# Three late tiles instead of four, part of the first ahead of the last split, and rounding work moved between engines

## The chip, the cores and the metric
The kernel runs on one core of a Trainium2 chip. The time is the device time of one execution in microseconds, the median of several runs. Lower is better.

## The reference, cut to what matters
```python
# 1. decayed linear attention over r, k, v (2 x 8 x 768 x 48), y -> x of 1536 tokens x 384
cur = einsum(u * kt, vt); y[t] = rt . (state + cur); state = w * state + einsum(kt, vt)
# 2. mixture of 8 experts, capacity 384, tokens kept in their order
expert_idx = argmax(x @ w_gate)                  # one expert for each token
disp[e, counts[e]] = x[i]; counts[e] += 1        # only while counts[e] < capacity
out[i] = gate_w[i] * (relu(disp @ w1[e]) @ w2[e])[pos[i]]
# 3. h = out @ w_in; softmax-weighted h, layer norm over 1024, @ w_out
```
All of it is float32. Products are made of parts: an operand is rounded to a high part (fp32r) and the remainder is its low part, so `w1_hi`, `w1_lo`, `xe_hi`, `xe_lo` exist beside the raw values.

## The kernel before, in words
The work is cut into tiles of 128 tokens, 12 of them (`NT`). A loop over the tiles does the attention; each turn t also splits tile t-1 into rows of x and logits (`split_x`, `take_logits`, `take_x`), picks each token's expert (`pick_experts`) and counts the tokens of each expert ahead of it (`count_before`), from which a slot in the table `x_slots` in DRAM follows (`place_tokens`). The tiles are picked in groups (`GROUPS`): 0-2, 3-5, 6-7, and then 8, 9, 10 and 11 alone. GpSimd scatters the rows of a tile to their slots with an indirect DMA (`scatter`, L566).

The first expert's rows are wanted before the last tiles could go through DRAM. So the tiles in `LATE` (8 to 11 before) are placed by TensorE: a 0/1 matrix `columns_of` says which token of the tile stands in which of the 224 slots of expert 0 (`rank_late`, `late_columns`, L1125 to L1137), and `place_late` (L1575) multiplies the tile's rows with it, three products of 224 columns, one for each third c of the 384 features, into three PSUM banks. The scattered tiles' rows of expert 0 are read back by SyncE (`load_rows(0, 0)`, L471, once all scatters of the tiles ahead of `LATE[0]` have landed) and turned into the same banks by `place_first_rows` (L1583). From the banks ScalarE rounds `xe_hi` (`act_first_xe_hi`) and VectorE takes the remainder `xe_lo` (`dve_first_xe_lo`, L963). Then the eight experts follow: `pe_up` (w1, eight blocks f, each needs its quarter of `w1_hi` and `w1_lo`), `pe_down` (w2), and between them sums and roundings of h on ScalarE and VectorE (L738, L969, L745, L976). After them come the last two matrix products with the norm.

The engines run in parallel and meet in semaphores; each works through its own list in the order in which the code issues it, and the code's order is written by hand. VectorE's list around the change is, in words: the end of the tile loop, counts and columns of the late tiles, quarters 1 and 2 of `w1_lo` (`lo_w1`, L522), `xe_lo`, and then L1199 to L1226, some fifteen small steps that find each token's place in the output (`sorted_to`). Only after them comes the first sum of h (L969). Quarter 3 of `w1_lo` is GpSimd's (L650), which waits for `sorted_ready` (L1226) first.

GpSimd's loop has, in each turn t, `last_keys(t + 1)` (L589), the decayed state (L619), `own_parts(t + 1)` (L577, L581) and then up to two scatters. VectorE's `add_own` (L1036) waits for `own_parts`.

Of the kernel before, what the change touches and what calls it, by code (L numbers as in the profile page):

```python
# [13 lines left out]
P = 128  # L14


def decay_attention_moe_solu(nc, r, k, v, w, u, w_gate, w1, w2, w_in, w_out, g_ln, out, CAP, N1):
# [27 lines left out]
    with ExitStack() as ctx:  # L45
# [107 lines left out]

        LATE = [NT - 4, NT - 3, NT - 2, NT - 1]
        columns_of = h[:].rearrange("p f n -> p (f n)")[:, 0:len(LATE) * N1].rearrange("p (t n) -> p t n", t=len(LATE))
# [261 lines left out]
        def _(sp):  # L417
# [14 lines left out]
            def load_first_w1(a):  # L432
                rows = slice(a, a + 1)
                sp.dma_start(w1_raw[:, 0, rows], w1_v[0][:, rows]).then_inc(usual.w1_in[0], 16)
# [16 lines left out]
            load_tile(9)  # L451
            load_first_w1(0)
            load_tile(10)
            load_first_w1(1)
            load_tile(11)
            load_first_w1(2)
            load_w2(0, 0)
# [75 lines left out]
        def _(pool):  # L533
# [73 lines left out]
            for t in range(1, NT):  # L607
# [18 lines left out]
                for _ in range(2):  # L626
                    if t >= GROUPS[group_of(stored)][-1] + 4:
                        if stored == 0:
                            pool.wait_ge(slots_zeroed, 16 * E)
                        scatter(stored)  # L630
                        stored += 1
# [116 lines left out]
        def _(act):  # L748
# [64 lines left out]
            for t in range(NT):  # L813
                if t > 0:
                    take_y(t - 1)
                    put_diagonal(t, 1)

                if t == NC:
                    take_k(t + 1)
                if t > 0:  # L820
                    take_x(t - 1)
                if t < NT - 1:
                    if t != NC:
                        take_k(t + 1)
                    put_diagonal(t + 1, 0)
                for n, g in enumerate(GROUPS):
                    if t == g[-1] + 2:
                        gate_exp(n)
                if t >= NT - 2:
                    act_w1_hi(act, 0, usual.w1_in[0], w1_loads(0, 1), usual.w1_hi, parts=[t - NT + 2])  # L830
            take_last_y()
            gate_exp(len(GROUPS) - 2)
            act_w1_hi(act, 0, usual.w1_in[0], w1_loads(0, 1), usual.w1_hi, parts=[2])
            take_x(NT - 1)
            act_w1_hi(act, 0, usual.w1_in[0], w1_loads(0, 1), usual.w1_hi, parts=[3])
            gate_exp(len(GROUPS) - 1)
            act_w2_hi(act, 0, usual.w2_in[0], 16, usual.w2_hi, parts=[0, 1])
            act_first_xe_hi(act)
            act_w2_hi(act, 0, usual.w2_in[0], 16, usual.w2_hi, parts=[2])

# [145 lines left out]
        def _(dve):  # L986
# [169 lines left out]
            for t in range(NT):  # L1156
# [15 lines left out]
                for n, g in enumerate(GROUPS):  # L1172
                    if t == g[-1] + 1:
                        pick_experts(n)
                    if t == g[-1] + 2:
                        if g[-1] in LATE:
                            rank_late(LATE.index(g[-1]))
                        else:
                            place_tokens(n)
                        add_picked(n)  # L1180
                        if g[-1] == LATE[0]:
                            late_columns(0)
            late_columns(1)
            rank_late(2)
            add_picked(len(GROUPS) - 2)
            take_logits(NT - 1)
            pick_experts(len(GROUPS) - 1)
            late_columns(2)
            rank_late(3)
            late_columns(3)  # L1190
            below_max(NT - 1)
            late_slots()
            add_picked(len(GROUPS) - 1)

            lo_w1(dve, 0, 0, usual, parts=[1, 2])
            dve_first_xe_lo(dve)

# [253 lines left out]
        def _(pe):  # L1451
# [122 lines left out]

            def place_late(j):  # L1575

                pe.wait_ge(columns_ready, j + 1)
                pe.wait_ge(x_ready, LATE[j] + 1)
                for c in range(KD):
                    pe.matmul(first_turned(c), x_rows(LATE[j])[:, c * P:(c + 1) * P], columns_of[:, j].bitcast(F32),  # L1580
                              start=(j == 0), stop=False, skip_group_check=True)

            def place_first_rows():  # L1583

                for m in range(usual.tiles):
                    pe.wait_ge(usual.rows_loaded[0][m], 16)
                for c in range(KD):
                    for m, rows in enumerate(usual.rows):
                        last = pe.matmul(first_turned(c)[:, m * P:m * P + rows], rows_in[0:rows, 0, m, c * P:(c + 1) * P],
                                         ident[0:rows, 0:rows], start=False, stop=(m == 1), skip_group_check=True)  # L1590
                    last.then_inc(usual.xe_turned, 1)

# [11 lines left out]
            for t in range(NT):  # L1604
# [8 lines left out]
                for n, g in enumerate(GROUPS):  # L1613
                    if t == g[-1] + 2:
                        count_before(n)
                chunk_out(b, t, c)
            count_before(len(GROUPS) - 2)
            split_x(NT - 1)
            place_late(0)
            place_late(1)  # L1620
            count_before(len(GROUPS) - 1)
            place_late(2)
            place_late(3)
            place_first_rows()
            pe.wait_ge(sum_ready, len(GROUPS))
# [117 lines left out]
```

## Time and profile before
| | us |
|---|---|
| time, median of 3 runs (lowest, highest) | 328.25 (327.98, 329.58) |
| the profiled execution's own time | 328.55 |
| its span, from first to last instruction | 326.8 |
| TensorE busy in it | 312.0 (95%) |
| VectorE busy | 212.2 (65%) |
| ScalarE busy | 196.1 (60%) |
| GpSimd busy | 188.5 (58%) |

The span has three parts: the attention with its tile loop up to about 74 us, the eight experts up to about 206 us, and the norm with the output. The change touches the end of the first and the start of the second. Durations below come from the profiled execution. Matmul records of float32 come in pairs (two passes), so three products of `place_late` are six records.

### The profile page before, as it was taken

The page shows a single profiled execution, that of the slowest core. Times are in us where ns is not written, and L with a number is a line of the kernel's source. Part 1 is how long each engine was busy: PE and PEld are TensorE (multiplying, and loading weights), DVE is VectorE, ACT ScalarE, POOL GpSimd, SP SyncE. Part 2 cuts the span into 40 slices and gives each one's busy share as a digit, 9 for nine tenths or more (in the row PEclk, how much of TensorE's full clock was granted, in tenths as well). Part 3 has the DMA queues.
Part 4 walks back from the last instruction along what each step waited for, and adds up shares of the span by engine and source line. Part 5 has one row for each costly group of instructions (what it writes and reads, how often), then busy time and mean ns, then how long its engine had stood idle before and what let it go on. Part 6 is the DMA issues. An engine that isn't in the chain of part 4 may idle for free.

```text
span 326.8 us, 6597 instructions
## 1 busy us (share of the span) xinstructions
PE 312.0 (95%) x2384; PEld 282.1 (86%) x2384; DVE 212.2 (65%) x489; ACT 196.1 (60%) x375; POOL 188.5 (58%) x170
## 2 busy tenths in 40 slices
PE   6799999989999999999999999999999999999991
PEld 3588888878999999999999999888999999999991
DVE  6856777897765647464555546898987676655610
ACT  2377786877667676676676767466565544543520
POOL 5985688761798898989898969501031101111221
PEclk9999999999999999999999999999999999999997
DMA  8999999971498949485757576000010000000010
GB/s 138 153 245 241 217 195 231 318 281 49 151 386 300 330 136 311 148 284 177 252 196 235 202 228 248 3 1 1 2 48 12 14 24 26 24 25 26 24 48 28
DMA packets 61650, 48.68 MB, mean 149 GB/s; under 512 B 42544, under 2 KB 57008, under 8 KB 61616
## 3 DMA queue, kind: packets, MB, share of 16 engines
q1 hardware_dynamic: 57856, 43.28, 46.0%
q0 software_dynamic: 1920, 4.73, 4.0%
q10 hardware_dynamic: 1840, 0.21, 0.9%
q8 instruction: 21, 0.34, 0.5%
q14 instruction: 13, 0.11, 0.1%
HBM read 38.37 MB, written 9.85 MB: 148 GB/s over the span
## 4 chain that ended last, share of the span: by engine, by line
PE 81%; DVE 6%; ACT 5%; issue 3%; DMA 1%; POOL 1%; DVEq 0%; ACTq 0%; POOLq 0%
PE ps L1391 24%; PE ps L1674 15%; PE ps L1657 15%; PE ps L1392 11%; PE ps L1683 3%; ACT scores L778 3%; PE ps L1527 2%; PE ps L1549 2%; PE ps L1495 2%; PE ps L1580 1%; DMA u_all<-in_u_dram 1%; PE ps L1464 1%; PE ps L1385 1%; PE ps L1522 1%; DVE scores L1054 1%
## 5 line engine op out<-in xcount | busy, mean ns | idle before, releaser
L522 POOL TENSOR_TENSOR w_lo<-w_raw,w_hi 128x768 fp32r<-128x768 f32 x33 | 60.5, 1860 | 9.9 <-DVE w_lo L528 9.8
L1391 PE MATMUL ps<-h,w_hi 128*128 128x448 f32 x192 | 61.8, 378 | 0.2 <-ACT h L745 0.2
L1391 PE MATMUL ps<-xe,w_hi 128*128 128x448 f32 x192 | 61.7, 377 | 0.3
L1674 PE MATMUL ps<-w_hi,h 128*128 128x384 f32 x192 | 51.4, 339 | 0.0
L1392 PE MATMUL ps<-xe,w_lo 128*128 128x224 f32 x192 | 50.7, 264 | 0.0
L1392 PE MATMUL ps<-h,w_lo 128*128 128x224 f32 x192 | 50.7, 264 | 0.0
L684 POOL TENSOR_TENSOR rstd<-var_b,minus_half 128x1 f32<-128x1 f32 x12 | 6.8, 565 | 71.3 <-DVE var_b L1337 71.3
L1657 PE MATMUL ps<-w_hi,xe 128*128 128x512 f32 x144 | 46.5, 392 | 0.2 <-DVE xe L1229 0.2
L969 DVE TENSOR_TENSOR ps<-ps,rk_in 128x448 f32<-128x448 f32 x32 | 20.2, 633 | 32.9 <-ACT rk_in L738 32.6
L1391 PEld LDWEIGHTS ps<-xe,w_hi 128*128 128x128 f32 x192 | 36.0, 188 | 5.0 <-issue 2.3
L528 POOL TENSOR_TENSOR w_lo<-w_raw,w_hi 128x1024 fp32r<-128x1024 f32 x16 | 38.2, 2408 | 1.5 <-DVE w_lo L528 1.5
L1391 PEld LDWEIGHTS ps<-h,w_hi 128*128 128x128 f32 x192 | 36.0, 188 | 3.1 <-ACT h L745 0.5
L1392 PEld LDWEIGHTS ps<-h,w_lo 128*128 128x128 f32 x192 | 36.6, 191 | 0.0
L1392 PEld LDWEIGHTS ps<-xe,w_lo 128*128 128x128 f32 x192 | 36.6, 191 | 0.0
L1674 PEld LDWEIGHTS ps<-w_hi,h 128*128 128x128 f32 x192 | 34.9, 188 | 0.0
L1657 PEld LDWEIGHTS ps<-w_hi,xe 128*128 128x128 f32 x144 | 27.0, 188 | 6.2 <-issue 0.7
L778 ACT ACTIVATE scores<-ident,own 128x128 f32<-128x128 f32 x92 | 29.3, 390 | 4.8 <-DVE own L1036 4.1
L1674 PE MATMUL ps<-w_lo,h 128*128 128x384 f32 x96 | 32.1, 335 | 0.0
L734 ACT ACTIVATE w_hi<-w_raw 128x1024 fp32r<-128x1024 f32 x24 | 24.6, 1055 | 8.6 <-PE ps L1392 7.3
L728 ACT ACTIVATE w_hi<-w_raw 128x768 fp32r<-128x768 f32 x36 | 29.4, 839 | 0.0
L1657 PE MATMUL ps<-w_lo,xe 128*128 128x512 f32 x72 | 28.1, 391 | 0.0
L745 ACT ACTIVATE h<-ps 128x448 fp32r<-128x448 f32 x32 | 17.4, 545 | 16.9 <-DVE ps L969 16.2
(166 smaller groups left out, 621.6 us busy)
## 6 DMA issues: line engine op xcount, KB each, us to landing
w_raw<-in_moe_w_dram SPq DMA_DIRECT2D x15, 1536.0 KB, 8.8
x_slots<-zeros SPq DMA_DIRECT2D x8, 336.0 KB, 4.3
rk_in<-in_r_dram SPq DMA_DIRECT2D x12, 192.0 KB, 4.4
rk_in<-in_k_dram SPq DMA_DIRECT2D x12, 192.0 KB, 4.8
v_in<-in_v_dram SPq DMA_DIRECT2D x12, 192.0 KB, 4.9
out_dram<-zeros SPq DMA_DIRECT2D x1, 2304.0 KB, 8.1
w_raw<-in_moe_w_dram SPq DMA_DIRECT2D x3, 512.0 KB
rows_in<-x_slots SPq DMA_DIRECT2D x8, 192.0 KB, 7.6
```

The source lines that it names most:

```text
L522: eng.tensor_tensor(w1_lo[:, :, cols], w1_raw[:, i, :, cols], w1_hi[:, :, cols].bitcast(F32), ALU.subtract).then_inc(g.w1_lo, 1)
L528: eng.tensor_tensor(w2_lo[:, :, cols], w2_raw[:, i, :, cols], w2_hi[:, :, cols].bitcast(F32), ALU.subtract).then_inc(g.w2_lo if d == 0 els ...
L728: act.activation(w1_hi[:, :, cols], w1_raw[:, i, :, cols], ACT.Copy).then_inc(hi_sem, 1)
L734: act.activation(w2_hi[:, :, cols], w2_raw[:, i, :, cols], ACT.Copy).then_inc(hi_sem, 1)
L745: act.activation(hi[:, 2 * j:2 * j + 2], first_sums(j, n), ACT.Relu).then_inc(g.h_hi, 1)
L778: last = act.activation(scores[:, t % 2, a, p, :], ident[:], ACT.Copy, scale=own[:, 2 * p + a:2 * p + a + 1])
L969: dve.tensor_tensor(first_sums(j, g.n), first_sums(j, g.n), h_rest[:, j % 2, :, 0:g.n], ALU.add)\
L1391: pe.matmul(ps[:, bank, 0:2 * n], w_hi, x[:, c, 0:2 * n], start=first, stop=False, skip_group_check=True)
L1392: return pe.matmul(ps[:, bank, 0:n], w_lo, x[:, c, 0:n], start=False, stop=last, skip_group_check=True)
L1657: last = pe.matmul(hidden_banks(t)[:, a, :], xt[:, c, i * P:(i + 1) * P], wt[:, c, a * 512:(a + 1) * 512], start=(c == 0 and z == 0), stop ...
L1674: last = pe.matmul(ps[:, OB + i, 0:DM], ht[:, f, i * P:(i + 1) * P], wt[:, f, :], start=(f == 0 and z == 0), stop=(f == KF - 1 and z == 2))
L1683: last = pe.transpose(ps[:, TB + f // 4, (f % 4) * P:(f % 4 + 1) * P], solu[i][:, f * P:(f + 1) * P], ident[:])
```

## The change
`LATE` loses tile 8, which is scattered like the ones ahead of it. To keep its scatter from coming too late, GpSimd scatters the tiles from 3 on one turn earlier. On TensorE two of the three products of the first late tile (now 9) stand ahead of the last count and `split_x(11)`; the third product and the rows from DRAM stand behind `split_x(11)`, and the last count and tiles 10 and 11 after them; so the last product into each bank is now one of `place_late(2)`, which releases `xe_hi`. On ScalarE the roundings of w1 and w2 change places with other work. On VectorE `late_columns` and `pick_experts` are reordered, `xe_lo` stands ahead of the two quarters of `w1_lo`, and `below_max(11)` behind them. SyncE issues thirds 1 and 2 of expert 0's w1 ahead of the loads of tiles 10 and 11.

```diff
-        LATE = [NT - 4, NT - 3, NT - 2, NT - 1]
+        LATE = [NT - 3, NT - 2, NT - 1]
@@ sync
             load_first_w1(0)
+            load_first_w1(1)
             load_tile(10)
-            load_first_w1(1)
+            load_first_w1(2)
             load_tile(11)
-            load_first_w1(2)
@@ gpsimd, in the tile loop
-                    if t >= GROUPS[group_of(stored)][-1] + 4:
+                    if stored < LATE[0] and t >= GROUPS[group_of(stored)][-1] + (3 if stored >= 3 else 4):
@@ scalar, in the tile loop: ahead of take_x, not at the turn's end
+                if t >= NT - 2:
+                    act_w1_hi(act, 0, usual.w1_in[0], w1_loads(0, 1), usual.w1_hi, parts=[t - NT + 2])
...
@@ scalar, behind the loop
+            act_w2_hi(act, 0, usual.w2_in[0], 16, usual.w2_hi, parts=[0])
+            act_first_xe_hi(act)
+            act_w2_hi(act, 0, usual.w2_in[0], 16, usual.w2_hi, parts=[1, 2])
             gate_exp(len(GROUPS) - 1)
-            act_w2_hi(act, 0, usual.w2_in[0], 16, usual.w2_hi, parts=[0, 1])
-            act_first_xe_hi(act)
-            act_w2_hi(act, 0, usual.w2_in[0], 16, usual.w2_hi, parts=[2])
@@ vector
-                    if t == g[-1] + 1:
+                    if t == g[-1] + 1 and t < NT - 1:
                         pick_experts(n)
...
+            pick_experts(len(GROUPS) - 2)
+            rank_late(1)
+            add_picked(len(GROUPS) - 2)
             late_columns(1)
...
-
+            dve_first_xe_lo(dve)
             lo_w1(dve, 0, 0, usual, parts=[1, 2])
-            dve_first_xe_lo(dve)
+            below_max(NT - 1)
@@ tensor
-            def place_late(j):
+            def place_late(j, parts=range(KD)):
...
+
+            place_late(0, range(2))
             count_before(len(GROUPS) - 2)
             split_x(NT - 1)
-            place_late(0)
+            place_late(0, range(2, KD))
+            place_first_rows()
+            count_before(len(GROUPS) - 1)
             place_late(1)
-            count_before(len(GROUPS) - 1)
             place_late(2)
-            place_late(3)
-            place_first_rows()
```

TensorE, from the end of the tile loop to the first expert, before. L1565/L1567 are the counts, L1549 `split_x`, L1580 `place_late`, L1589 the rows from DRAM:

```order
L1565 MATMUL ps<-picked,tri_bf 128x8 [waits picked_ready,state_ready,late_rank,sum_ready]
L1549 MATMUL ps<-pick_pair,yt 128x104 [waits x_ready,even_pairs_ready]
L1580 MATMUL ps<-h,w_raw 128x224 [waits x_ready,columns_ready]
L1580 MATMUL ps<-h,w_raw 128x224 x2
L1565 MATMUL ps<-picked,tri_bf 128x8 [waits picked_ready,state_ready,late_rank,sum_ready]
L1580 MATMUL ps<-h,w_raw 128x224 [waits x_ready,columns_ready]
L1580 MATMUL ps<-h,w_raw 128x224 x2
L1589 MATMUL ps<-ident,rows_in 128x128 [waits usual_rows_loaded01,usual_rows_loaded00]
L1627 MATMUL ps<-picked_sum,ones_bf 128x8 [waits late_rank,sum_ready]
```

And of the change (L1563 is the count, L1547 `split_x`, L1578 `place_late`):

```order
L1578 MATMUL ps<-h,w_raw 128x224 [waits x_ready,columns_ready]
L1578 MATMUL ps<-h,w_raw 128x224
L1563 MATMUL ps<-picked,tri_bf 128x8 [waits picked_ready,state_ready,late_rank,sum_ready]
L1547 MATMUL ps<-pick_pair,yt 128x104 [waits x_ready,even_pairs_ready]
L1578 MATMUL ps<-h,w_raw 128x224 [waits x_ready,columns_ready]
L1589 MATMUL ps<-ident,rows_in 128x128 [waits usual_rows_loaded01,usual_rows_loaded00]
L1563 MATMUL ps<-picked,tri_bf 128x8 [waits picked_ready,state_ready,late_rank,sum_ready]
L1578 MATMUL ps<-h,w_raw 128x224 [waits x_ready,columns_ready]
L1578 MATMUL ps<-h,w_raw 128x224 x2
L1627 MATMUL ps<-picked_sum,ones_bf 128x8 [waits late_rank,sum_ready]
```

Two products now stand ahead of the count, and one late tile is gone: before, two tiles stood on each side of the second count, each as a pair of rows (rows that only repeat are left out).

VectorE, just ahead of the steps that find each token's place (L522 is `w1_lo`, L963 `xe_lo`, L1075 `below_max`):

```order
+L963 TENSOR_TENSOR xe<-ps,xe 128x224 [waits usual_xe_hi] x3
+L522 TENSOR_TENSOR w_lo<-w_raw,w_hi 128x3x256 [waits usual_w1_hi] x2
 L1075 TENSOR_SCALAR below<-logits,lmax 128x8
-L1141 TENSOR_SCALAR slot_b<-rank 128x4
-L1143 SCALAR_TENSOR_TENSOR slot<-slot_a,slot_b 128x4 [waits late_slot_a]
-L1151 TENSOR_REDUCE picked_sum<-picked 128x8 [waits counts_done,picked_ready]
-L522 TENSOR_TENSOR w_lo<-w_raw,w_hi 128x3x256 [waits usual_w1_hi] x2
-L963 TENSOR_TENSOR xe<-ps,xe 128x224 [waits usual_xe_hi] x3
-L1199 TENSOR_SCALAR kept<-ps 128x8 [waits total_done]
```

The two quarters of `w1_lo` change sides with `xe_lo`; L1199 is the first step of the chain to `sorted_to`, which now follows L1075.

GpSimd, turns 8 to 10 of the tile loop (L566 is a scatter):

```order
+L566 DMA x_slots<-place,slot 3072x384 [waits x_ready,slot_ready] x2
 L589 TENSOR_TENSOR place<-rk_in,wlast 128x8x48 [waits update_done,k_turned,loaded2]
 L619 TENSOR_TENSOR place<-place,wsq 128x256 [waits y_done,state_ready]
 L577 TENSOR_TENSOR own_place<-rk_in,u_all 128x384 [waits own_step,loaded2,picked_ready]
 L581 TENSOR_TENSOR own_place<-own_place,rk_in 128x384 [waits own_ready,own_step]
-L566 DMA x_slots<-place,slot 3072x384 [waits x_ready,slot_ready] x2
+L566 DMA x_slots<-place,slot 3072x384 [waits x_ready,slot_ready]
```

The scatters of tiles 3 and 4 now stand ahead of the work for tile 10, and one scatter (tile 5) stands where two did.

## Rows read from the trace of the kernel before
**Rows 1.** The page, part 1: busy time, share of the span.
```profile
PE 312.0 (95%) x2384; PEld 282.1 (86%) x2384; DVE 212.2 (65%) x489; ACT 196.1 (60%) x375; POOL 188.5 (58%) x170
```
**Rows 2.** Busy time by stretch, PE alone: window, PE busy (records), clock, DMA share, GB/s.
```profile
74.20:81.40 7.20, 7.17 (x48) 1.00 0.15 47
81.40:90.30 8.90, 8.64 (x53) 1.00 0.48 155
90.30:205.00 114.70, 114.45 (x735) 1.00 0.71 244
```
**Rows 3.** Chain that ended last: start us, us, what.
```profile
84.17 0.55 ACT rk_in L738
...
89.71 0.52 ACT h L745
...
90.31 0.44 PE ps L1391
```
**Rows 4.** Timeline, PE: start us, us, engine line op, tiles, count [idle before].
```profile
74.22 1.14 PE L1549 MATMUL ps<-pick_pair,yt 128*128 128x104 f32 x8
75.20 2.46 PE L1580 MATMUL ps<-h,w_raw 128*128 128x224 f32 x12
...
77.55 2.52 PE L1580 MATMUL ps<-h,w_raw 128*128 128x224 f32 x12
79.90 1.47 PE L1589 MATMUL ps<-ident,rows_in 128*128 128x128 f32 x12
81.21 0.17 PE L1627 MATMUL ps<-picked_sum,ones_bf 128*128 128x8 bf16 x1
```
**Rows 5.** Timeline, DVE, end of the routing.
```profile
79.24 1.84 DVE L522 TENSOR_TENSOR w_lo<-w_raw,w_hi 128x768 fp32r<-128x768 f32 x2
...
82.11 0.16 DVE L1199 TENSOR_SCALAR kept<-ps 128x8 f32<-128x8 f32 x1
...
83.37 0.44 DVE L1217 TENSOR_SCALAR token<-expsum 128x12 f32<-128x12 f32 x1
...
84.36 0.17 DVE L1226 TENSOR_TENSOR sorted_to<-place_a,place_c 128x12 int32<-128x12 f32 x1
84.82 0.63 DVE L969 TENSOR_TENSOR ps<-ps,rk_in 128x448 f32<-128x448 f32 x1 [0.29 <-issue]
```
**Rows 6.** Timeline, POOL, turn 9 on.
```profile
58.61 1.01 POOL L577 TENSOR_TENSOR own_place<-rk_in,u_all 128x384 f32<-128x384 f32 x1 [0.73 <-DVE picked L1103]
59.70 1.01 POOL L581 TENSOR_TENSOR own_place<-own_place,rk_in 128x384 f32<-128x384 f32 x1
60.85 1.01 POOL L566 DMA_INDIRECT x_slots<-place,slot  x1
62.16 0.98 POOL L566 DMA_INDIRECT x_slots<-place,slot  x1 [0.30 <-issue]
...
70.51 0.97 POOL L566 DMA_INDIRECT x_slots<-w_raw,slot  x1 [0.30 <-issue]
...
85.09 1.89 POOL L522 TENSOR_TENSOR w_lo<-w_raw,w_hi 128x768 fp32r<-128x768 f32 x1
```
**Rows 7.** Timeline, DVE, turns 10 and 11.
```profile
61.80 0.55 DVE L1036 TENSOR_REDUCE own<-own_place 128x8 f32<-128x384 f32 x1
...
63.61 0.83 DVE L1084 SCALAR_TENSOR_TENSOR lscore<-logits,lmax,desc 128x8 f32<-128x8 f32 x1
...
72.94 0.23 DVE L1084 SCALAR_TENSOR_TENSOR lscore<-logits,lmax,desc 128x8 f32<-128x8 f32 x1
```
**Rows 8.** Timeline, the queue of SyncE.
```profile
73.12 14.41 SPq L466 DMA_DIRECT2D rows_in<-x_slots  x4
```
**Rows 9.** DMA issues of 70 to 86 us: count, KB each, us to landing.
```profile
rows_in<-x_slots SPq DMA_DIRECT2D x1, 192.0 KB, 2.5
```
**Rows 10.** Timeline, ACT, turn 10 (w1_hi, then the last y but one).
```profile
69.22 0.83 ACT L728 ACTIVATE w_hi<-w_raw 128x768 fp32r<-128x768 f32 x1
69.95 0.57 ACT L791 ACTIVATE yt<-ps 128x512 f32<-128x512 f32 x1
```

More of the change, by code:

```diff
@@ L828, in _ @@
                         gate_exp(n)
-                if t >= NT - 2:
-                    act_w1_hi(act, 0, usual.w1_in[0], w1_loads(0, 1), usual.w1_hi, parts=[t - NT + 2])
             take_last_y()
@@ L1177, in _ @@
                             rank_late(LATE.index(g[-1]))
+                            late_columns(LATE.index(g[-1]))
                         else:
@@ L1180, in _ @@
                         add_picked(n)
-                        if g[-1] == LATE[0]:
-                            late_columns(0)
+            pick_experts(len(GROUPS) - 2)
+            rank_late(1)
+            add_picked(len(GROUPS) - 2)
             late_columns(1)
-            rank_late(2)
-            add_picked(len(GROUPS) - 2)
             take_logits(NT - 1)
             pick_experts(len(GROUPS) - 1)
+            rank_late(2)
             late_columns(2)
-            rank_late(3)
-            late_columns(3)
-            below_max(NT - 1)
             late_slots()
             add_picked(len(GROUPS) - 1)
+            dve_first_xe_lo(dve)
             lo_w1(dve, 0, 0, usual, parts=[1, 2])
-            dve_first_xe_lo(dve)
+            below_max(NT - 1)
             dve.wait_ge(total_done, 1)
@@ L1573, in count_before @@
                 last.then_inc(counts_done, 1)
-            def place_late(j):
+            def place_late(j, parts=range(KD)):
                 pe.wait_ge(columns_ready, j + 1)
                 pe.wait_ge(x_ready, LATE[j] + 1)
-                for c in range(KD):
-                    pe.matmul(first_turned(c), x_rows(LATE[j])[:, c * P:(c + 1) * P], columns_of[:, j].bitcast(F32),
-                              start=(j == 0), stop=False, skip_group_check=True)
+                for c in parts:
+                    last = pe.matmul(first_turned(c), x_rows(LATE[j])[:, c * P:(c + 1) * P], columns_of[:, j].bitcast(F32),
+                                     start=(j == 0), stop=(j == len(LATE) - 1), skip_group_check=True)
+                    if j == len(LATE) - 1:
+                        last.then_inc(usual.xe_turned, 1)
             def place_first_rows():
@@ L1588, in place_first_rows @@
                     for m, rows in enumerate(usual.rows):
-                        last = pe.matmul(first_turned(c)[:, m * P:m * P + rows], rows_in[0:rows, 0, m, c * P:(c + 1) * P],
-                                         ident[0:rows, 0:rows], start=False, stop=(m == 1), skip_group_check=True)
-                    last.then_inc(usual.xe_turned, 1)
+                        pe.matmul(first_turned(c)[:, m * P:m * P + rows], rows_in[0:rows, 0, m, c * P:(c + 1) * P],
+                                  ident[0:rows, 0:rows], start=False, stop=False, skip_group_check=True)
             pe.wait_ge(zero_ready, 1)
```

## The prediction
> **What bounds the kernel now.** I read the page's busy times first: TensorE is busy for 312.0 of 326.8 us [rows 1]. Then the busy time by stretch: from 74.2 to 81.4 us TensorE is busy for 7.17 of 7.20 us, from 90.3 to 205 for 114.45 of 114.70 [rows 2]. Work taken off its list in the first stretch shortens the kernel if nothing else is late. In between, from 81.4 to 90.3 us, the chain of waits leaves TensorE: it runs over ScalarE's L738 at 84.17, VectorE, ScalarE's L745 at 89.71, and is back on TensorE only at 90.31, in the middle of the first `pe_down` [rows 3]. The reader is to see that TensorE is full on both sides of this, while the chain between is one of VectorE and ScalarE. From 90.31 on I let a shift pass through unchanged. So the question is when the first sum of h (L969, at 84.82 [rows 5]) starts, not when `pe_up` does: from L969 to TensorE's row at 90.31 it is 5.49 us, in an order that the change does not touch.
>
> **TensorE's list.** The 24 records of `place_late` take 77.49 - 75.20 = 2.29 us for two tiles and 79.90 - 77.55 = 2.35 for the other two [rows 4] (the count sits at 77.49), 0.19 a record. A tile is 6 records, 1.16 us: removed. Two thirds of the next, 4 records, 0.77 us: moved ahead of `split_x(11)`. Together 1.93 us less between `split_x(11)`, at 74.22, and L1627, at 81.21 [rows 4]. The moved records stand where TensorE waited for little: its last row of the loop ends near 73.7, so they end near 74.5 and `split_x(11)` slips by some 0.3 us, if the loop ends when it did.
>
> **What happens ahead of it.** ScalarE's rounding of a quarter of w1 goes from 69.22, right ahead of the y at 69.95 for which TensorE waits [rows 10], to a place where ScalarE waits for logits. That takes up to 0.73 us out of one wait. But GpSimd's list changes too. The scatters of tiles 3 and 4 (60.85 and 62.16, two that take 2.45 us with the gaps [rows 6]) now stand ahead of the work for tile 10. GpSimd ran without a gap up to there, but L577 waited 0.73 us for the picks, to 58.61 [rows 6]. So it is 2.45 - 0.73 = 1.7 us late, and L581, over at 60.71, is over at 62.4. VectorE's L1036, which waits for it, began at 61.80 [rows 7]. It waits 0.6 us, and for three quarters of a turn VectorE's list has no slack. Of these 0.6 us a part returns: one row of L1084 takes 0.83 us and a later one 0.23 [rows 7], the first beside a GpSimd operation, and the columns of the first late tile leave turn 10. The next turn I put at +0.1 us. With the 0.3 above, `split_x(11)` starts at about 74.65, +0.43 us.
>
> A sentence from the Trainium skill, SBUF — State Buffer, section Who interferes with whom: VectorE and GpSimd share one port pair, an exclusive lock, and whoever starts first holds it for its whole instruction. The long L1084 agrees. By that rule the sum would move with every new overlap, in both directions, by at most one such row at a time, and I change nothing for it.
>
> **The scatter of tile 8 and the rows.** The last scatter ahead of the rows began at 70.51 [rows 6], and the rows were issued at 73.12 [rows 8], each landing in 2.5 us [rows 9]: about 75.6 and 76.0. Now the queue on GpSimd is one scatter longer but begins a turn earlier; I count L581 of tile 11 ending at 67.5, two scatters, the state, and tile 8's scatter at 70.8: +0.3, rows in at 76.3. TensorE reaches them at 74.65 + 0.98 (L1549) + 0.38 (the third product) = 76.0, where it used to reach them at 79.90 [rows 4]. Cover of 3.9 us is gone; what is left is a wait of 0 to 0.3 us, I take 0.1. The wait stands ahead of the last count and both last tiles, so all of it would count.
>
> Then L1627 comes at 81.21 + 0.43 - 1.93 + 0.10 = 79.8. `pe_up` can start about 1.4 us earlier. Its fillers: the columns of the last tile are ready at about `split_x(11)` + 3.8 us and TensorE is there at + 3.9.
>
> **VectorE's list, where the gain goes.** Before, `w1_lo` (two of 0.92 us, 79.24 to 81.08) ran while the rows were turned, and `xe_lo` followed, done at 82.11 when L1199 began [rows 5]. Now `xe_lo` comes first and VectorE idles until `xe_hi` is there. `xe_lo` ends at 82.11 - 1.40 + 0.1 (the last record is one of 224 columns) = 80.8. Behind it come 1.84 us of `w1_lo` and 0.1 of `below_max`, then L1199 to L1226, which took 84.53 - 82.11 = 2.42 us. In them L1217 took 0.44 us beside a scatter [rows 5]; the late scatters are one fewer and start as early, so they should be over by 83, and I take 0.28 off: 2.14. L969 may start at 80.8 + 1.84 + 0.1 + 2.14 + 0.05 = 84.95, against 84.82. Without that credit it is 85.2, with no shift of `split_x(11)` 84.5.
>
> So L969 moves by +0.15 us (-0.3 to +0.8), although `pe_up` starts 1.4 us sooner. TensorE gives its lead back twice: at block 6, whose `w1_lo` is GpSimd's row of 1.89 us (85.09 before [rows 6]) and again waits for `sorted_ready`, now due at 84.9, so that block 6 can start at 86.85 and not at about 85.9; and in `pe_down`, at 90.45.
>
> SyncE's order costs nothing: w1's thirds come sooner, the loads of tiles 10 and 11 wait behind 0.5 MB each, and they have over 5 us until use. ScalarE's two quarters of w2 behind `xe_hi` (about 2.0 us) end at 82.5, ahead of its first row of h at 84.17 before [rows 3]; were they late, VectorE would not notice before 84.5. The exp of tile 11 waits for `below_max`, at 82.8, done before it is read.
>
> **Sum.** The profiled execution took 328.55 us, 326.8 of span and 1.75 around it; +0.15 makes 328.7. The median before is 0.3 below that execution, so I say 328.4.
>
> **The rivals.**
> *The lead survives* (faster in tendency). If the time were set by TensorE's list and not by L969, -1.93 + 0.43 + 0.1 = -1.4 us: 326.9. For it speaks that TensorE is full from 74 to 81. Against it that the chain leaves TensorE at 84.17, and VectorE's 1.94 us of rounding and comparing now stand directly in that chain. Chance 0.14.
> *The earlier scatters cost nothing upstream.* If GpSimd keeps up in turn 9, or VectorE catches up, `split_x(11)` starts at 74.2, L969 at 84.5, -0.3: 328.0. For it: ScalarE's move takes 0.73 us out of a wait on the same way. Chance 0.22.
> *The rows land late* (slower). The one mechanism: TensorE stands at the first row from DRAM. Place: behind the third product of tile 9. Every microsecond that they land after 76.0 is a microsecond of the end. The point from which it makes the kernel slower than before is a landing about 0.1 us later than I assume, and it leaves the band of 0.5% at about 1.5 us. One more scatter turn (1.31 us) on GpSimd, or SyncE's issue slipping behind an unfinished scatter, gives +1.3 on my +0.15: 329.7; a landing twice as slow as the 2.5 us gives +2.5: 330.9. Against it: the scatters queued are as many per stretch. Chance 0.14.
> *The forecast itself*, L969 bound, +0.15: chance 0.50, its own range 328.0 to 329.0.
>
> **Range and chances.** A measurement of this kernel can tell about 0.5%, 1.6 us, from no change: faster is under 326.6, slower over 329.9. The range takes in the surviving lead and the late rows up to one scatter: 326.9 to 329.8. Faster 0.06, same 0.86, slower 0.08.
>
> **What would show it.** In the changed profile: TensorE's first L1391 row about 1.4 us earlier, near 80.2; a wait of VectorE ahead of `xe_lo`; TensorE idle for 0.7 to 1 us at block 6 of the first `pe_up`, and for about 1 us in the first `pe_down`; L969 within 0.5 us of 84.82. L1036 of tile 10 waiting for L581 shows the upstream step, TensorE's wait at L1589 the rows. I am wrong if L969 comes before 84 or if TensorE stands more than 0.5 us at L1589.

## The result, and the profile after

| | median of 6 | lowest to highest | profiled execution (span) |
|---|---|---|---|
| before | 328.21 us | 327.98 to 329.58 | 328.55 (326.8) |
| changed | 329.90 us | 329.46 to 330.44 | 329.46 (327.6) |

The ratio is 1.0047, with an interval of 1.0028 to 1.0066. The kernel became slower by more than the runs scatter, and by slightly less than the 0.5% that the forecast called no change. I had forecast 328.4, with a range of 326.9 to 329.8: the median lies 0.1 us above the range, and the ratio applied to the 328.25 from which I had worked, 329.8, at its upper edge.

Part 1 of the page of the changed kernel (busy time, share, records), then the busy time of TensorE in three stretches that answer to [rows 2] (window, busy, clock, DMA share, GB/s):

```profile
PE 312.1 (95%) x2376; PEld 281.4 (86%) x2378; DVE 211.1 (64%) x490; ACT 196.4 (60%) x375; POOL 188.5 (58%) x170
```
```profile
74.20:81.20 7.00, 6.55 (x46) 1.00 0.17 53
81.20:90.30 9.10, 8.45 (x52) 1.00 0.43 135
90.30:205.00 114.70, 113.82 (x731) 1.00 0.71 243
```

The clock granted to TensorE is full (1.00, 2.4 GHz) in all three, as before, so the clock is no part of the difference between these two profiles. TensorE now idles 0.45 us ahead of the first expert where it idled 0.03, 0.65 in the next stretch where it idled 0.26, and 0.88 in the third where it idled 0.25. The timeline of TensorE shows both places (start us, us, line, tiles, count, idle before; L1563 counts, L1547 is `split_x`, L1578 `place_late`, L1389 and L1390 the products of an expert):

```profile
73.19 1.09 PE L1525 MATMUL ps<-scores,v_in 128*64 128x128 f32 x16 [1.10 <-DVE scores L1054]
74.21 1.02 PE L1578 MATMUL ps<-h,w_raw 128*128 128x224 f32 x4
...
75.23 1.11 PE L1547 MATMUL ps<-pick_pair,yt 128*128 128x104 f32 x8
76.18 0.56 PE L1578 MATMUL ps<-h,w_raw 128*128 128x224 f32 x2
77.00 1.55 PE L1589 MATMUL ps<-ident,rows_in 128*128 128x128 f32 x12 [0.25 <-DMA rows_in<-x_slots]
...
78.44 2.52 PE L1578 MATMUL ps<-h,w_raw 128*128 128x224 f32 x12
80.79 0.17 PE L1627 MATMUL ps<-picked_sum,ones_bf 128*128 128x8 bf16 x1
81.16 0.44 PE L1389 MATMUL ps<-xe,w_hi 128*128 128x448 f32 x1 [0.20 <-DVE xe L963]
...
87.81 0.44 PE L1389 MATMUL ps<-xe,w_hi 128*128 128x448 f32 x1 [0.65 <-POOL w_lo L522]
...
91.19 0.44 PE L1389 MATMUL ps<-h,w_hi 128*128 128x448 f32 x1 [0.65 <-ACT h L745]
```

`pe_up` starts at 81.16, half a microsecond ahead of before (81.66), and `split_x(11)` at 75.23, a microsecond behind [rows 4]. The lead is lost at block 6 (87.81), and the first `pe_down` waits as well. The chain of waits says through what the time ran (start us, us, what):

```profile
70.92 2.62 DMA x_slots<-w_raw,slot
73.56 0.34 SPq L466
...
73.94 2.92 DMA rows_in<-x_slots
...
77.00 1.55 PE ps L1589 x12
78.58 1.63 PE ps L1578 x8
80.23 0.36 ACT xe L722
80.62 1.15 DVE xe L963 x3
81.77 1.73 DVE w_lo L522 x2
...
85.71 0.64 DVE ps L969
```

Before, the chain came from TensorE's list and left it only at 84.17 [rows 3]. Now it comes from the last scatter and the rows from DRAM, crosses TensorE, and is on VectorE from 80.62 on. L969 starts at 85.71, against 84.82 [rows 5].

**A yardstick.** GpSimd's last store of the output, in the changed kernel:

```profile
321.61 0.97 POOL L688 DMA_INDIRECT out_dram<-v_in,of_row  x1 [3.19 <-ACT v_in L914]
```

It starts 235.90 us behind L969. In the kernel before it starts at 320.77, 235.95 us behind. In the twelve profiles of this study the distance lies between 235.9 and 236.2, so the start of the first L969 tells what a change ahead of it is worth, free of what varies behind it. What varies ahead of it from one execution to the next is still in it, and each run has one profile. All runs, with the differences from before in us (the timed one is the ratio less one times 328.5; for "changed" and each run against the kernel before on its own chip):

| kernel | `split_x(11)` | first row of L1589 | L969 | L969 less 84.82 | timed |
|---|---|---|---|---|---|
| before | 74.22 | 79.90 | 84.82 | | |
| changed | 75.23 | 77.00 | 85.71 | +0.89 | +1.5 (0.9 to 2.2) |
| the same again | 76.30 | 78.39 | 87.11 | +2.29 | +1.1 (0.6 to 1.7) |
| old scatter rule | 74.49 | 77.41 | 86.13 | +1.31 | +1.7 (1.1 to 2.3) |
| `w1_lo` first | 75.05 | 76.83 | 85.02 | +0.20 | +0.5 (0.0 to 0.9) |
| `w1_lo` in the wait | 75.36 | 76.97 | 84.81 | -0.01 | +0.6 (0.1 to 1.1) |
| tile 8 not waited for | 75.14 | 76.71 | 85.42 | +0.60 | +0.5 (0.1 to 1.0) |
| quarter 0 behind the mask | 74.22 | 76.58 | 85.30 | +0.48 | +1.1 (0.6 to 1.7) |
| w1 behind the rows | 75.24 | 76.98 | 85.70 | +0.88 | +1.2 (0.7 to 1.7) |
| four late, waits filled | 73.71 | 79.21 | 83.81 | -1.01 | -0.4 (-0.9 to +0.1) |
| quarter 0 in the count's wait | 74.07 | 79.30 | 84.10 | -0.72 | -0.9 (-1.4 to -0.4) |
| two thirds ahead, alone | 74.57 | 80.09 | 84.70 | -0.12 | +0.2 (-0.3 to +0.6) |

Executions of every kernel here, the one before included, fall into two groups about 1.1 us apart; the profile of "the same again" is the only one from the upper group, and it is 1.15 us late at the first count, near 51 us, because the clock granted to TensorE was 0.50 (1.2 GHz) from 16 to 19 us there, so that +2.29 is to be read as +1.14:

```profile
16.00:17.00 1.00, 1.00 (x12) 0.50 1.33 167
```

### The profile page after: what moved, and what is told of

It is laid out like the page before. It is cut to its first block, busy times and chain, and to the rows that moved or that the text cites. A ratio compares the mean times of both kernels' runs of the same rounds, so it can differ in the third digit from the quotient of the medians.

```text
span 327.6 us, 6584 instructions
## 1 busy us (share of the span) xinstructions
PE 312.1 (95%) x2376; PEld 281.4 (86%) x2378; DVE 211.1 (64%) x490; ACT 196.4 (60%) x375; POOL 188.5 (58%) x170
## 4 chain that ended last, share of the span: by engine, by line
PE 73%; DVE 8%; ACT 6%; issue 5%; POOL 3%; DMA 3%; SPq 0%; DVEq 0%; POOLq 0%; ACTq 0%
PE ps L1389 23%; PE ps L1674 15%; PE ps L1657 15%; PE ps L1390 11%; ACT scores L778 4%; PE ps L1683 3%; PE ps L1383 1%; DVE own L1036 1%; DMA wsq<-in_w_dram 1%; PE ps L1525 1%; DVE place L994 1%; DMA rows_in<-x_slots 1%; ACT yt L791 1%; DMA x_slots<-w_raw,slot 1%; POOL own_place L577 1%
## 5 line engine op out<-in xcount | busy, mean ns | idle before, releaser
L522 POOL TENSOR_TENSOR w_lo<-w_raw,w_hi 128x768 fp32r<-128x768 f32 x33 | 60.3, 1852 | 11.2 <-DVE w_lo L528 9.9
L1389 PE MATMUL ps<-xe,w_hi 128*128 128x448 f32 x192 | 61.9, 378 | 1.1 <-POOL w_lo L522 0.7
L1389 PE MATMUL ps<-h,w_hi 128*128 128x448 f32 x192 | 61.8, 377 | 0.6 <-ACT h L745 0.6
L1390 PE MATMUL ps<-h,w_lo 128*128 128x224 f32 x192 | 50.8, 265 | 0.0
L1390 PE MATMUL ps<-xe,w_lo 128*128 128x224 f32 x192 | 50.8, 264 | 0.0
L969 DVE TENSOR_TENSOR ps<-ps,rk_in 128x448 f32<-128x448 f32 x32 | 20.2, 632 | 32.8 <-ACT rk_in L738 32.8
L1389 PEld LDWEIGHTS ps<-xe,w_hi 128*128 128x128 f32 x192 | 36.0, 187 | 5.8 <-issue 3.1
L1389 PEld LDWEIGHTS ps<-h,w_hi 128*128 128x128 f32 x192 | 36.0, 188 | 3.6 <-ACT h L745 0.9
L1390 PEld LDWEIGHTS ps<-h,w_lo 128*128 128x128 f32 x192 | 36.6, 191 | 0.0
L1390 PEld LDWEIGHTS ps<-xe,w_lo 128*128 128x128 f32 x192 | 36.6, 191 | 0.0
```

Source lines behind the costliest of these rows:

```text
L522: eng.tensor_tensor(w1_lo[:, :, cols], w1_raw[:, i, :, cols], w1_hi[:, :, cols].bitcast(F32), ALU.subtract).then_inc(g.w1_lo, 1)
L969: dve.tensor_tensor(first_sums(j, g.n), first_sums(j, g.n), h_rest[:, j % 2, :, 0:g.n], ALU.add)\
L1389: pe.matmul(ps[:, bank, 0:2 * n], w_hi, x[:, c, 0:2 * n], start=first, stop=False, skip_group_check=True)
L1390: return pe.matmul(ps[:, bank, 0:n], w_lo, x[:, c, 0:n], start=False, stop=last, skip_group_check=True)
```

## The experiments

**The old scatter rule.** Do the earlier scatters push `split_x(11)` back, and would it help to undo them?

```diff
-                    if stored < LATE[0] and t >= GROUPS[group_of(stored)][-1] + (3 if stored >= 3 else 4):
+                    if t >= GROUPS[group_of(stored)][-1] + 4:
```

> The changed kernel with GpSimd's old scatter rule (four turns behind the group for every tile, so tile 8's scatter comes last, behind tiles 6 and 7). Reference points of the changed kernel: L1036 of tile 10 at 62.49 after a wait of 0.48 us for L581, split_x(11) at 75.23, rows landed at 76.86, L1589 at 77.00, L969 at 85.71, median 329.9. Theory U (the earlier scatters delay VectorE in turn 10 and that delay is what costs): L1036 waits no more, split_x(11) comes 0.5 to 0.9 us earlier, and the time falls by as much, to 329.0 to 329.4. Theory R (the rows from DRAM now end the wait, whatever stands ahead): the last scatter starts at about 71.8 instead of 70.92, the rows land 0.9 us later, L1589 starts near 77.9 although split_x(11) is earlier, and the time rises by 0.5 to 0.9 us to about 330.6. I expect R in its price and U in its first step.

```profile
77.41 1.55 PE L1589 MATMUL ps<-ident,rows_in 128*128 128x128 f32 x12 [1.41 <-DMA rows_in<-x_slots]
```

L1036 of tile 10 no longer waited (61.90), and `split_x(11)` came 0.74 us sooner. So 0.74 us of the slip of 1.01 is the scatters' price. But the last scatter began at 71.80 instead of 70.92, TensorE stood 1.41 us at the rows, and L969 was 0.42 later than in the changed kernel. The time is 330.28 us, ratio 1.0052, no better than the changed kernel's. The rows from DRAM gate TensorE there.

**`w1_lo` ahead of `xe_lo`.** Is it VectorE's order that turns TensorE's lead into nothing?

```diff
-            dve_first_xe_lo(dve)
-            lo_w1(dve, 0, 0, usual, parts=[1, 2])
             below_max(NT - 1)
+            lo_w1(dve, 0, 0, usual, parts=[1, 2])
+            dve_first_xe_lo(dve)
```

> The changed kernel with VectorE's tail in the order of before: below_max(11), two quarters of w1_lo, then xe_lo. Theory V (the start of L969 at the end of VectorE's list sets the time, and TensorE's list does not): w1_lo fills the 0.55 us in which VectorE waited for xe_hi, pe_up starts later by about 1.1 us (82.3 instead of 81.16), yet L969 comes 0.5 us earlier (85.2) and the time falls by 0.5 us to 329.4. Rival T (the start of pe_up sets the time): the time rises by 1.1 us to 331.0.

```profile
82.22 0.44 PE L1389 MATMUL ps<-xe,w_hi 128*128 128x448 f32 x1 [1.20 <-DVE xe L963]
...
85.02 0.63 DVE L969 TENSOR_TENSOR ps<-ps,rk_in 128x448 f32<-128x448 f32 x1
```

`pe_up` starts 1.06 us later than in the changed kernel, and L969 0.69 earlier. Had TensorE's list set the end, this kernel would have been slower than the changed one by a microsecond. It was not (ratio 1.0014, 1.0000 to 1.0027). That refutes the rival of the surviving lead.

**`w1_lo` in VectorE's wait.** The changed kernel's VectorE waits 1.23 us for the last count, just ahead of where its list becomes the path. One quarter of `w1_lo` goes there, which takes it out of the path.

```diff
             pick_experts(len(GROUPS) - 1)
+            lo_w1(dve, 0, 0, usual, parts=[1])
...
             dve_first_xe_lo(dve)
-            lo_w1(dve, 0, 0, usual, parts=[1, 2])
+            lo_w1(dve, 0, 0, usual, parts=[2])
```

> The changed kernel with quarter 1 of w1_lo (0.91 us) moved into the 1.23 us in which VectorE waits for the last count, behind pick_experts(6); quarter 2 stays behind xe_lo. Theory V (VectorE's list sets the time): sorted_to and L969 come 0.9 us earlier (L969 at 84.8), TensorE's two stalls at block 6 and in pe_down shrink by 0.6 to 0.9 us, and the time falls by 0.9 us to 329.0. Rival T (start of pe_up): no change, 329.9. Rival: the quarter runs over the end of the wait and delays the last columns; then TensorE would stand ahead of place_late(2) and the gain is 0.5 us or less.

VectorE in this kernel, around that wait:

```profile
77.53 0.95 DVE L522 TENSOR_TENSOR w_lo<-w_raw,w_hi 128x768 fp32r<-128x768 f32 x1
78.70 0.17 DVE L1125 CUSTOM_DVE_ANT_0 rank_e<-ps,picked 128x8 f32<-128x8 f32 x1 [0.22 <-PE ps L1566]
...
84.81 0.63 DVE L969 TENSOR_TENSOR ps<-ps,rk_in 128x448 f32<-128x448 f32 x1
```

The wait shrank from 1.23 to 0.22 us, L969 came 0.90 earlier, and block 6 no longer waited; the first `pe_down` still did, for 0.62 us, at 90.30. A microsecond off VectorE's list between `xe_lo` and L969 is a microsecond of L969: the mechanism of the forecast. The timed difference stayed at +0.6, though, where the yardstick says nothing is left.

**Rows that do not wait for tile 8's scatter.** The rows are read once tiles 0 to 7 are scattered, and tile 8 is scattered with the late tiles. This kernel leaves the tokens of tile 8 out of expert 0.

```diff
-            sp.wait_ge(scattered, 16 * LATE[0])
+            sp.wait_ge(scattered, 16 * (LATE[0] - 1))
@@ gpsimd
-                    if stored < LATE[0] and t >= GROUPS[group_of(stored)][-1] + (3 if stored >= 3 else 4):
+                    if stored < LATE[0] - 1 and t >= GROUPS[group_of(stored)][-1] + (3 if stored >= 3 else 4):
...
-            for t in LATE:
+            for t in [LATE[0] - 1, *LATE]:
```

> The changed kernel, but tile 8 is scattered with the late tiles, behind the load of expert 0's rows, and the load waits for tiles 0 to 7 only. This leaves the tokens of tile 8 out of expert 0; all engines do the same work otherwise. Theory R (the landing of the rows is on the path): the last scatter ahead of the rows starts at 69.13 instead of 70.92, the rows land near 75.2, TensorE's wait of 0.4 us at L1589 goes, L969 comes 0.4 us earlier, and the time falls by 0.4 us in the profile; if the timed executions wait longer there than the profiled one did (their medians lie 0.4 us above it), by up to 0.9 us, to 329.0, with a smaller spread over the runs (0.98 us in the changed kernel). Rival (rows were not on the path): no change, 329.9.

The last scatter ahead now began at 69.12, 1.8 us sooner, but the rows were issued at 73.45, only 0.11 sooner: from its start to the issue that scatter took 4.33 us. The DMA engines were still full (share 0.99 to 1.0) for its first 0.9 us; that the weights held it up is my reading, and the run does not isolate it. The wait at L1587 was still there, L969 moved by -0.29, and the run does not separate the two theories of the rows.

**The change again, quarter 0 behind the mask, w1 behind the rows.** Three kernels. The first repeats the changed kernel unaltered. The second takes VectorE's quarter 0 of `w1_lo`, which the changed kernel runs between the two halves of the last masking while TensorE waits 1.10 us, and puts it behind `pick_experts(5)`. The third loads expert 1's w1 behind the rows, so that no weights are in the DMA queues (their share is 0 from 67 to 69 us).

```diff
-                    if t == NT - 1 and a == 1:
-                        lo_w1(dve, 0, 0, usual, parts=[0])
...
+            lo_w1(dve, 0, 0, usual, parts=[0])
```

> The changed kernel itself once more, unaltered, so that its relatives have it on the same chip. In its first runs it stood at 1.0047 of the time before while its one profiled execution, the fastest of six, had L969 only 0.89 us later. Both theories (VectorE's list sets the time; TensorE's does) expect 1.003 to 1.006 here. If the landing of the rows varies between executions, as I suppose, this kernel's executions spread by about 1 us where those of before lie within 0.3 us, and a second profile shows another start of L1589.

> The changed kernel with quarter 0 of w1_lo (0.86 us) taken out from between VectorE's two last maskings (L1054) and put behind pick_experts(5), where VectorE waits 0.52 us for a count. TensorE waited 1.10 us for the second masking. Theory R (the landing of the rows is on the path, so what stands ahead of it no longer counts): split_x(11) comes 0.8 us earlier, near 74.4, the rows still land near 76.9, TensorE's idle time at L1589 grows from about 0.4 to 1.2 us, L969 stays at 85.7 and the time stays as that of the changed kernel (ratio to it 0.999 to 1.001). Rival U (the upstream delay of VectorE is what costs): L969 and the time fall by 0.8 us.

> The changed kernel with the 1.5 MB load of expert 1's w1 issued behind the two loads of expert 0's rows, not ahead of them. Theory Q (the scatters land late since they queue behind the weights, with which the DMA engines are full until 70.5 us): the DMA share falls below 1 some 4 us sooner, the scatter of tile 8 lands within 1.6 to 2 us of its start at 70.9 instead of 2.64, the rows are issued near 72.7 and land near 75.6, TensorE's wait at L1589 goes, and the time falls by 0.4 us in the profile and up to 1 us in the timed executions, which then spread less. Rival (the latency of the scatter is fixed): the rows are issued at 73.5 as before, no change. Expert 1's w1 is used from 88 us on, so its later load should cost nothing.

The rows in TensorE's timeline, of the three in this order:

```profile
78.39 1.55 PE L1589 MATMUL ps<-ident,rows_in 128*128 128x128 f32 x12 [0.58 <-DMA rows_in<-x_slots]
```
```profile
76.58 1.55 PE L1588 MATMUL ps<-ident,rows_in 128*128 128x128 f32 x12 [0.84 <-DMA rows_in<-x_slots]
```
```profile
76.98 1.55 PE L1589 MATMUL ps<-ident,rows_in 128*128 128x128 f32 x12 [0.23 <-DMA rows_in<-x_slots]
```

With quarter 0 away from the mask `split_x(11)` came 1.01 us earlier, but the rows were issued only 0.06 earlier (73.50), and TensorE's wait grew by 0.6. The 0.41 us that L969 gained are the landing's, which took 2.56 us here and 2.92 in the changed kernel, and not quarter 0's:

```profile
73.89 2.56 DMA rows_in<-x_slots
```

The ratio did not move (1.0035, as for the change again). With w1 out of the way the last scatter began at 71.01 and the rows were issued at 73.66: 2.65 us, as in the changed kernel (70.92 to 73.56, 2.64) and before (70.51 to 73.12, 2.61 [rows 6, 8]). My theory of the queues missed: what is left in them is not what makes the rows late in the changed kernel's profile. The change again had 2.96 us between the two (72.08 to 75.04), and another landing, so this way through DRAM varies by some 0.3 us between executions of one kernel.

**Four late tiles, with the change's other moves.** If tile 8's scatter costs more than its 1.16 us of TensorE bring, the rest of the change may be worth more without it. To the kernel before: the two thirds ahead of the count, ScalarE's and SyncE's moves, and quarter 0 away from the mask, into the wait for the last logits. Three late tiles, the earlier scatters and VectorE's new order are left out. TensorE's part of the edit:

```diff
+            place_late(0, range(2))
             count_before(len(GROUPS) - 2)
             split_x(NT - 1)
-            place_late(0)
+            place_late(0, range(2, KD))
```

> The kernel before (four late tiles, old scatter rule, rows last, w1_lo quarters 1 and 2 ahead of xe_lo) with only those edits of the change that do not lean on the rows: two thirds of the first late tile ahead of the last count but one, ScalarE's roundings ahead of take_x, one w2 rounding behind xe_hi, w1's thirds issued earlier; and quarter 0 of w1_lo taken from between the maskings into the wait for the last logits. By my theory (VectorE's list ahead of L969 sets the time, and the rows only count where TensorE meets them early): split_x(11) near 73.8 instead of 74.22, L1627 near 80.0 instead of 81.21, L1589 starts without a wait near 78.7, xe_lo is done near 80.9 instead of 82.1, L969 near 83.6 instead of 84.82, and the time is 1.2 us below that of before (327.0 where before has 328.2). Rival (every gain on TensorE ahead of the experts is given back, whatever is done on VectorE): within 0.3 us of before.

VectorE and ScalarE in this kernel:

```profile
78.36 1.81 DVE L522 TENSOR_TENSOR w_lo<-w_raw,w_hi 128x768 fp32r<-128x768 f32 x2
80.21 1.28 DVE L963 TENSOR_TENSOR xe<-ps,xe 128x224 fp32r<-128x224 f32 x3
...
83.81 0.63 DVE L969 TENSOR_TENSOR ps<-ps,rk_in 128x448 f32<-128x448 f32 x1 [0.17 <-ACT rk_in L738]
```
```profile
83.17 0.55 ACT L738 ACTIVATE rk_in<-ps 128x448 f32<-128x448 f32 x1 [0.20 <-PE ps L1391]
```

`pe_up` started at 80.75 and L969 at 83.81, a microsecond ahead of before. Here L969 waits for ScalarE, and ScalarE for TensorE: with VectorE's old order the path is TensorE's list again. The timed gain is 0.4 us, where I had expected 1.2, and not clear of zero. Which of the moves brought it is not taken apart.

**Quarter 0 in the wait for the count.** The same, with quarter 0 a little earlier in VectorE's list, in its wait of 0.66 us for the count.

```diff
             late_columns(1)
+            lo_w1(dve, 0, 0, usual, parts=[0])
             rank_late(2)
             add_picked(len(GROUPS) - 2)
-            lo_w1(dve, 0, 0, usual, parts=[0])
             take_logits(NT - 1)
```

> As b3_four_late_fill_waits, but quarter 0 of w1_lo stands where VectorE waited 0.66 us for a count (behind the columns of the second late tile, ahead of rank_late(2)) and no longer ahead of the last logits, which then come 0.5 us sooner. In the profiles so far the last store of the kernel started 235.9 to 236.04 us after the first L969 whatever was changed ahead of it, so L969 is the yardstick. Theory V: L969 goes from 83.81 to about 83.3, the last store from 319.85 to 319.3, and the time is 1.0 to 1.5 us below before on the yardstick; the medians may show 0.3 us less of it than the yardstick, as they did for b3. Rival: TensorE (rows of the first expert at 80.75, block 6 and GpSimd's quarter) is the limit by now, no change against b3.

```profile
84.10 0.63 DVE L969 TENSOR_TENSOR ps<-ps,rk_in 128x448 f32<-128x448 f32 x1 [0.37 <-issue]
```

327.98 us, ratio 0.9973 (0.9958 to 0.9988): faster than both kernels. L969 is 0.29 later than in the run above, but so is the first count (51.02 against 50.71), 20 us ahead of the edit; counted from there the two are equal, so the further 0.5 us that I expected did not come. Whether this place is better than the last one stays open, as their intervals overlap.

**Two thirds ahead, alone.** The kernel before with the same TensorE edit, and quarter 1 of `w1_lo` in the wait for the last count instead of behind it.

> The kernel before with one part of the change alone, two thirds of the first late tile ahead of the last count but one, and quarter 1 of w1_lo in VectorE's 0.89 us wait for the last count. Four late tiles, old scatter rule, ScalarE and SyncE as before. Theory V: TensorE's L1627 comes 0.4 us earlier (80.8), VectorE's xe_lo is done at 81.7 instead of 82.1, L969 at 84.4 instead of 84.82, the time 0.4 us below before. Rival (the move itself costs, since split_x(11) slips by 0.3 us and picks and counts with it): no gain or 0.3 us slower.

TensorE and VectorE in this kernel:

```profile
77.33 2.92 PE L1581 MATMUL ps<-h,w_raw 128*128 128x224 f32 x12
80.09 1.47 PE L1590 MATMUL ps<-ident,rows_in 128*128 128x128 f32 x12
```
```profile
77.19 0.95 DVE L522 TENSOR_TENSOR w_lo<-w_raw,w_hi 128x768 fp32r<-128x768 f32 x1
78.06 0.16 DVE L1125 CUSTOM_DVE_ANT_0 rank_e<-ps,picked 128x8 f32<-128x8 f32 x1
...
81.34 1.04 DVE L963 TENSOR_TENSOR xe<-ps,xe 128x224 fp32r<-128x224 f32 x3 [0.93 <-ACT xe L722]
```

My expectation missed. Before, VectorE waited 0.89 us for this count, which TensorE ran at 77.52. The moved records bring the count to 77.13, and VectorE reaches the place at 77.19: what is left of the wait is some 0.3 us, and the row of 0.95 overran it. The last columns came late, and TensorE stood inside L1581, whose twelve records took 2.92 us where they take 2.52. No gain (1.0005).

## Why the prediction was right in its mechanism and short in its size

**Right.** TensorE's list lost what was counted: from `split_x(11)` to L1627 it is 80.79 - 75.23 = 5.56 us, against 6.99, that is 1.43 less, and with the 0.4 us at the rows 1.8 of the 1.93. The lead of `pe_up` was 0.5 us and not 1.4, and it was given back at block 6 and in `pe_down`, where the prediction put it (87.81 and 91.19, waits of 0.65 each, forecast 0.7 to 1 us). From L969 to the row of `pe_down` behind that wait it is 5.48 us, against 5.49 before. L969 sets the time: "`w1_lo` first" and "`w1_lo` in the wait" showed it, by moving `pe_up` and L969 apart. From the end of `xe_lo`, 81.77, to L969 it is 3.94 us, where the terms gave 4.13. The credit of 0.28 us for L1217 (L1215 now, 0.18 us at 84.83) is in that, but by luck: the late scatters were not over by 83, the last ended at 84.75, 0.08 us ahead of the row. In "`w1_lo` first" the same row met one and took 0.46 us.

**Wrong: the term "`split_x(11)` starts at about 74.65, +0.43 us".** It measured +1.01: +0.57 at TensorE's last `scores` row (73.19, 72.62 before) and +0.44 from there, where I had put "the next turn at +0.1" and 0.3 for the moved records. VectorE in turns 9 (L1036), 10 (L1084) and 11, and the L1084 of turn 10 in the kernel before:

```profile
62.49 0.55 DVE L1036 TENSOR_REDUCE own<-own_place 128x8 f32<-128x384 f32 x1 [0.48 <-POOL own_place L581]
...
69.41 0.71 DVE L1084 SCALAR_TENSOR_TENSOR lscore<-logits,lmax,desc 128x8 f32<-128x8 f32 x1
...
70.84 0.73 DVE L1054 COPY_PREDICATED scores<-causal,ps 128x512 f32<-128x512 int32 x1
71.46 0.95 DVE L522 TENSOR_TENSOR w_lo<-w_raw,w_hi 128x768 fp32r<-128x768 f32 x1
72.32 0.72 DVE L1054 COPY_PREDICATED scores<-causal,ps 128x512 f32<-128x512 int32 x1
```
```profile
69.28 0.23 DVE L1084 SCALAR_TENSOR_TENSOR lscore<-logits,lmax,desc 128x8 f32<-128x8 f32 x1
```

L1036 waited for GpSimd and came 0.69 us late (forecast 0.6). By L1084 the slip was down to 0.13 (69.41 against 69.28), which is the return that I had counted on: the columns of the first late tile had left the turn. Then L1084 itself took 0.71 us instead of 0.23. Before, it started 0.08 us into a scatter (69.20) and was not held; now it started 0.28 us into one (69.13) and was. So the loss stood in a row of the very line that I had used to argue for a return, in a turn that I had not looked at: the 0.83 us of [rows 7] are turn 9's and are still 0.83 us in the changed kernel, the 0.23 turn 11's. I had quoted the rule for it, SBUF — State Buffer of the Trainium skill, Who interferes with whom, and had "changed nothing for it", taking such rows to fall out both ways. The trace agrees with its lock in so far as the row is held until the scatter is over (70.10).

Behind it came quarter 0, between the two maskings, ahead of the one for which TensorE waited 1.10 us. ScalarE's move, which I had left out of the sum, may have paid: `split_x(10)` came at 70.33 us against 70.58, in spite of the slip, and the wait for the masking swallowed it. With the old scatter rule `split_x(11)` came at 74.49, and with quarter 0 moved at 74.22: the scatters' order is worth 0.74 us of TensorE's arrival, the place of quarter 0 1.01.

**Too small: the wait at the rows.** I took 0.1 us of 0 to 0.3, without a reason: my own figures, rows in at 76.3 and TensorE there at 76.0, give 0.3. By 0.19 us a record the third product ends near 76.6, and L1589 starts at 77.00, so it was 0.4, and 0.8 in the change again (0.25 and 0.58 as the profile counts idle time), there beyond the 0.5 that I had named as proof against me. The scatter began at 70.92 (forecast 70.8) and the issue followed 2.64 us later, as before. The landing took 2.9 us for the second part, where I took 2.5 from [rows 9]:

```profile
rows_in<-x_slots SPq DMA_DIRECT2D x1, 192.0 KB, 2.4
rows_in<-x_slots SPq DMA_DIRECT2D x1, 144.0 KB, 2.9
```

The two terms also hide each other. TensorE starts L1589 at the later of its own arrival, 76.6, and the rows, 76.9. That is why taking away the scatters' price, or quarter 0's, did not make the kernel faster: it lengthened the wait. The rival of the late rows was this mechanism, at about a fourth of the 1.3 us that I gave it in this profile; and where that rival says that the kernel is slower than before only from a landing 0.1 us later, my own sum had it 0.15 slower already.

**The sum.** The end of `xe_lo` was forecast at 80.8 and came at 81.77, +0.97: 0.58 by `split_x(11)`, 0.3 by the rows, 0.1 by the last steps of TensorE. VectorE's list behind it took 0.19 less than I had counted. 0.15 + 0.97 - 0.19 is 0.93, against the measured 0.89 at L969, which is beyond the -0.3 to +0.8 that I had allowed. That is half of the miss in the time, 328.4 against 329.90. The other half is a term of its own: I set the median 0.3 us below the profiled execution, as it was before, and the changed kernel's median lies 0.44 above its profiled execution, which was the fastest of the six.

**Open.** The timed differences of the changed kernel, +1.5 and +1.1 us, lie above the 0.9 of the profiles, and so do those of several of its variants ("`w1_lo` in the wait": +0.6 against 0.0). The profile of the change again, in which TensorE waited longer at the rows, gives L969 10.81 us behind `split_x(11)`, where the first gives 10.48. In these two profiles the issue of the rows came 2.64 and 2.96 us behind the scatter. That such variation is the rest of the timed difference was not shown; no run here isolates it. Joining "`w1_lo` in the wait" to "quarter 0 behind the mask" was not tried; the rows at 76.6 bound what it could give.

## What to carry to other kernels

Look for the instruction behind which everything keeps a constant distance, and judge each edit by what it does to that one: the tensor engine was 95% busy here, and 1.9 us off its list bought nothing, because the vector engine's list between two waits had grown by as much. Moving the reader of a transfer forward spends its cover: the rows had 3.9 us of it, and from the moment it is gone every gain upstream only lengthens the wait. What did pay was putting work that must be done anyway into a wait longer than the work, and the wait has to be measured for that: 0.95 us of work in a wait of 1.23 brought L969 0.90 us sooner, and in a wait of 0.3 it cost what it was to save.

## What the runs showed of the hardware

From the start of GpSimd's last scatter ahead of the rows (128 rows of 1536 B) to the issue that waits for it, it is 2.60 to 2.65 us in eight of the twelve profiles, one of them with no weights queued beside it. In the other four it is 2.80 ("quarter 0 in the count's wait"), 2.96 (the change again), 3.79 ("four late, waits filled") and 4.33 ("tile 8 not waited for"). The Trainium skill, DMA: Bandwidth & Descriptors, section Anatomy of one DMA — SWDGE (gpsimd) path, gives some 2.0 us fixed plus the bytes by 436 GB/s; an estimate by it is 2.0 + 0.45 = 2.45 us, and the trace agrees within 0.2 in the eight. Its section Latency and other measured facts says that a lighter load on DRAM makes the fixed part smaller. The twelve profiles go that way: the mean busy share of the DMA engines in the first half microsecond of the scatter was 0.51 to 0.69 in the eight, and 0.70, 0.74, 0.80 and 1.0 in the four, in the order of their delays. Below that it bought nothing more: without weights, at 0.51, it is still 2.65 us. No run changed the load alone at the higher shares, so the order is seen and the cause not isolated.

Small rows of VectorE are held beside a scatter, but not by its start. L1084 of turn 10 (128 x 8) stands beside one in all twelve profiles: it took 0.23 us in the five where it began 0.08 to 0.16 us into it, and 0.71 to 0.74 in the seven where it began 0.26 to 0.28 us into it. (The five also stand beside the first scatter of a pair and the seven beside the second; L1089 of the kernel before took 0.45 us where it began 0.54 us into a first one, and 0.23 with none.) An edit that moves either engine by 0.2 us decides anew whether such a row costs 0.5.

TensorE's clock is not the same in every execution of one kernel: in the change again it was 1.2 GHz from 16 to 19 us, and the sixteen products of L1493 that start at 15.74 took 2.00 us where the changed kernel's took 1.16 at 2.4 GHz. TensorE had idled 1.8 us just before in both.
